# A mixer kernel on one core: TensorE's filler transposes ahead of the gated layer are taken out

## The reference, cut to what matters

```python
# attention, 4 x 8 heads, 576 x 64 each, causal, with a decaying bias
scores = scale * np.matmul(q, k.transpose(0, 1, 3, 2))
cum = np.cumsum(np.maximum(s, 0.0), axis=-1)
bias = -(cum[:, :, :, None] - cum[:, :, None, :])
scores = np.where(causal, -1e9, scores + np.minimum(bias, 0.0))
attn = softmax(scores);  x = attn @ v            # heads side by side: 576 x 512
# the gated layer: x mixed with x one token back
xk = mu_k * x + (1.0 - mu_k) * x_prev;  xr = mu_r * x + (1.0 - mu_r) * x_prev
k = np.maximum(xk @ w_k, 0.0);  v = k * k @ w_v
x = sigmoid(xr @ w_r) * v
# the mixer: over tokens, then over channels
h = np.maximum(x.T @ w_tok1, 0.0) @ w_tok2;  u = x + h.T
out = u + np.maximum(u @ w_ch1, 0.0) @ w_ch2
```

## Time and profile before

| | |
|---|---|
| median of 3 executions | 952.55 us (948.29 to 953.51) |
| the profiled execution: its own time | 947.21 us |
| its span, first to last instruction | 945.4 us |
| mean granted TensorE clock over the span | 0.987 |
| TensorE busy with matmuls | 888.6 us, 94% |
| VectorE, ScalarE, GpSimd busy | 55%, 41%, 42% |
| slots 0 to 33, up to the first product of the gated layer | about 128.5 us |

### The profile page before, as it was taken

How to read it: one execution, slowest core, us unless ns; L and a number is a source line. 1 busy time by engine, 2 the same in 40 slices (tenths; PEclk the granted TensorE clock), 3 DMA queues, 4 the chain that set the end, 5 groups by cost and what they waited for, 6 DMA issues and landing times.

```text
span 945.4 us, 18975 instructions
## 1 busy us (share of the span) xinstructions
PE 888.6 (94%) x6693; PEld 826.9 (87%) x6693; DVE 519.9 (55%) x1228; ACT 384.9 (41%) x985; POOL 396.4 (42%) x684
## 2 busy tenths in 40 slices
PE   5886789999999999999999989999999999999997
PEld 3665578889888988888899979999999999999996
DVE  3666668878878788787866743222323232323222
ACT  2575567566565666656634521211121112111110
POOL 4576986957778677776657327000000000000000
PEclk9997799999999999999999999999999999999999
DMA  7521212031320312212040240100010001000000
GB/s 243 141 85 38 64 39 64 20 95 38 89 59 24 95 39 81 61 32 70 2 184 27 76 151 9 51 26 1 25 50 25 0 25 50 25 0 26 1 26 26
DMA packets 79982, 51.62 MB, mean 55 GB/s; under 512 B 60321, under 2 KB 69089, under 8 KB 79905
## 3 DMA queue, kind: packets, MB, share of 16 engines
q1 hardware_dynamic: 79904, 50.63, 18.6%
HBM read 41.10 MB, written 9.51 MB: 54 GB/s over the span
## 4 chain that ended last, share of the span: by engine, by line
PE 72%; issue 8%; DVE 7%; POOL 6%; ACT 4%; DMA 1%; SPq 1%; DVEq 0%; POOLq 0%; ACTq 0%
PE psum L175 55%; PE psum L760 6%; PE psum L716 3%; PE psum L731 3%; POOL sq L641 2%; DVE z L1131 2%; ACT z L944 2%; POOL v_hl L564 1%; PE psum L697 1%; DVE p_t L1149 1%; PE psum L854 1%; POOL z L578 1%; POOL k_lo L645 1%; PE psum L741 1%; PE psum L834 1%
## 5 line engine op out<-in xcount | busy, mean ns | idle before, releaser
L175 PE MATMUL psum<-u_hi,c_hi 128*128 128x288 f32 x384 | 116.9, 304 | 2.8 <-DVE u_lo L1266 2.8
L1276 DVE SCALAR_TENSOR_TENSOR hid_lo<-psum,hid_hi 128x288 fp32r<-128x288 f32 x96 | 43.9, 457 | 132.7 <-ACT hid_hi L1050 132.7
L1050 ACT ACTIVATE hid_hi<-psum 128x288 fp32r<-128x288 f32 x96 | 39.4, 411 | 184.2 <-PE psum L175 184.2
L175 PE MATMUL psum<-hid_hi,c_hi 128*128 128x288 f32 x384 | 113.9, 297 | 0.0
L175 PE MATMUL psum<-u_hi,c_lo 128*128 128x288 f32 x384 | 113.7, 296 | 0.0
L175 PE MATMUL psum<-u_lo,c_hi 128*128 128x288 f32 x384 | 113.6, 296 | 0.0
L578 POOL TENSOR_SCALAR z<-cum_k,cum_qp 128x128 f32<-128x128 f32 (+4 forms) x160 | 91.7, 582 | 51.8 <-DMA cum_k<-cum_scratch 42.6
L175 PE MATMUL psum<-hid_hi,c_lo 128*128 128x288 f32 x384 | 113.3, 295 | 0.0
L175 PE MATMUL psum<-hid_lo,c_hi 128*128 128x288 f32 x384 | 113.2, 295 | 0.0
L944 ACT ACTIVATE z<-z,z_min 128x128 f32<-128x128 f32 (+4 forms) x160 | 95.1, 596 | 37.7 <-DVE z_min L1131 37.4
L1131 DVE CUSTOM_DVE_ANT_0 z<-psum,z 128x128 f32<-128x128 f32 (+4 forms) x160 | 70.5, 477 | 25.0 <-PE psum L716 17.8
(11 more groups left out here) (121 smaller groups left out, 2335.0 us busy)
## 6 DMA issues: line engine op xcount, KB each, us to landing
cum_k<-cum_scratch SPq DMA_DIRECT2D x32, 288.0 KB, 3.7
q_raw<-in_q SPq DMA_DIRECT2D x32, 144.0 KB, 2.6
k_raw<-in_k SPq DMA_DIRECT2D x32, 144.0 KB, 2.8
mixed_scratch<-gate SPq DMA_DIRECT2D x32, 144.0 KB, 1.8
x_t<-mixed_scratch SPq DMA_DIRECT2D x8, 576.0 KB, 4.4
out<-o_sb SPq DMA_DIRECT2D x24, 192.0 KB, 2.1
v_raw<-in_v SPq DMA_DIRECT2D x32, 128.0 KB, 2.5
c_raw<-in_moe_w_ch SPq DMA_DIRECT2D x4, 768.0 KB, 6.4
```

The costliest lines, as they stand in the source:

```text
L175: done = nc.tensor.matmul(out, w[a][0:r, tw, w_cols], x[b][0:r, tx, x_cols], start=first and n == 0 and m == 0, stop=last and n == len(til ...
L1050: nc.scalar.activation(hid[0][:, f % 3, :], s_bank[f % 2][:, 0:HALF], ACT.Relu).then_inc(hid_hi, 1)
L1276: nc.vector.scalar_tensor_tensor(hid[1][:, f % 3, :], s_bank[f % 2][:, 0:HALF], 0.0, hid[0][:, f % 3, :].bitcast(F32), ALU.max, ALU.subtra ...
```

## The change

One constant goes from 4 to 0. In slots 0 to 33 keep_busy() then issues nothing, so 34 times 4 transposes of 128 x 128 are gone from TensorE's list, with their weight loads. Everything else, on TensorE and on the other engines, keeps its order and its waits.

```diff
--- before.py
+++ after.py
@@ -67,7 +67,7 @@
 GATE_AT = 34
 FIRST_PAIRS, TURN_PAIRS = [0, 7, 14, 21], [-6, 4]
 PAIR_AT = FIRST_PAIRS + [GATE_AT + turn * TURN_SLOTS + at for turn in range(STEPS - 2) for at in TURN_PAIRS]
-KEEP = 4
+KEEP = 0
 LAST_SLOT = GATE_AT + STEPS * TURN_SLOTS
 TWO_LEFT = GATE_AT + (STEPS - 2) * TURN_SLOTS
 
```

## The result

The change makes the kernel slower. Its median is 963.34 us (961.28 to 967.04, 4 executions) against 950.42 (945.85 to 953.51, 4 executions); the ratio is 1.0152 with a 95% interval of 1.0114 to 1.0189. Later, in other executions beside other kernels, it was 1.0183 (1.0147 to 1.0220). The forecast of 953 and its range to 962 are both exceeded. These ratios are not the quotients of the two medians, which are 1.0136 and 1.0194.

The account below looks back on a forecast made before the run. TensorE's chain of waits and its clock were taken to bound the first 128.5 us: 4.4 us of filler back, 5.4 lost to a late first rise, +1.0 on the 952.55 median, forecast 953 us; range 946 to 962, 8 times in 10.

Parts of the forecast that it names:

- the chance of falls in the thin stretches: Between vA and w3, around q and k: perhaps a clock fall without filler; no separate price or chance.
- Rival (2): Slots 0 to 33: clock stays low for most of the stage, +18 us, 970.5; two late rises 960; chance 0.25.
- the filler's removal from the waits: Behind k, w4, s3 and w2: TensorE waits there anyway, so removing transposes costs and gives nothing; idle time becomes longer.
- The step on the first rise: Near 29 us, first pair of heads: the shortened unbroken run makes the clock rise late, costing 5.4 us from vA to vB.
- The price of the low level: First pair of heads at the lower clock: 5.4 us from vA to vB, plus 2.4 for its s-pieces.
- the filler's own time: Removed transposes on TensorE's chain up to 128.5 us: 4.4 us come back, at most 7.2, at least nothing.
- the gated layer's start: First product expected between 128 and 131 us; from there to the end the two traces should differ by nothing.
- The long x_mix of VectorE behind GpSimd's weights: 92.6 to 108 us: VectorE waits out GpSimd's weights, 2.36 us for one and 5.36 for two; no filler gain counted there.

## Why the prediction was wrong

**The step that failed is the chance of falls in the thin stretches.** Rival (2) named it ("perhaps a fall in the thinner stretch between vA and w3"), weighed it with "more than the 0.95 us in 4.0 ahead of a fall, but not by much", and gave it no price: its 22.4 us are all put down to late rises. The only falls in the trace of before had come behind nearly idle stretches, and I took these for the border. They were only examples on one side of it. The changed kernel lost its clock with 1.24 and with 1.84 us of work in 3.40; a stretch with 2.16 in 3.42 holds in the kernel before (and no new border lies between these: 2.35 fell and 1.76 held elsewhere, as shown above). What I had not done is to go through one pair and add up what is left in each wait without the filler: I had written that the filler's removal from the waits "costs and gives nothing; the idle time becomes longer", and it was exactly there that it did its work. Eight transposes at the two thinnest places alone give the time of before back (0.9987), with no filler left on the chain, though not its clock (0.964 to 0.976 over the span, against 0.977 to 0.985).

**The step on the first rise was the wrong one to forecast.** I expected it late, at 5.4 us, as the one loss. In the profiled execution it came close to 28.0 us, within an unbroken run of 4.8 us; in the other one it was missed behind a run just as long and came some 28 us later. So that it "can go either way" was right, and the mechanism exists, but the two executions lie at 962 and 967 us, not at 948 and 953.

**The price of the low level was nearly right.** The prediction's pieces make 5.4 + 2.4 = 7.8 us for one pair. Measured, a pair at the low level takes 28.6 us and one at the high level 21.1, so 7.5. In part that is luck: vB takes 2.1 us more at the low level (4.4 against 2.3), not 1.6, and s1 (1.65 against 0.96) was left out, while the wait ahead of k becomes 0.5 us shorter. By the granted clocks of the two windows up to the gated layer (0.68 of 145.92 and 0.92 of 128.53 us) the changed kernel was at the low level for some 73 us more, two and a half pairs; an estimate from these numbers is 19 us, less what the filler's own time gives back, against the 17.4 measured. The +7 to +18 us of rival (2) are where the result lies, and I had given that rival 0.25; but its price was of late rises, and that falls in the thin stretches come to as much is luck too.

**The filler's own time was put too high.** 4.4 us on the chain by the prediction; 2.6 and about 2 by the two pairs of kernels that differ in nothing else, with intervals that overlap. (The prediction also counts one piece too many behind w1: three of 0.44 us stand in the chain, at 49.07, 70.30 and 126.73. Its sum doesn't use them.) The chain of waits counts a piece in full if it was the last thing before the next. The rows of the kernel with no filler between vA and q show where the rest went: q starts earlier, but the wait between q and k grows to 1.08 us, because ScalarE isn't free for q_t any sooner (it is at the low part o_lo until 31.11 and begins q_t at 31.14). From vA to k it is 3.41 us there (32.19 - 28.78), before 3.61 by the same two rows; 0.2 of the 0.46 us came back.

**What held.** Nothing changed behind the gated layer's start but 2.4 us made up, which no run took apart. The long x_mix of VectorE behind GpSimd's weights is there in both kernels and isn't most of the loss: in the changed kernel

```profile
78.45 4.28 DVE L1202 SCALAR_TENSOR_TENSOR x_mix<-x_all,mu,x_mix 128x288 f32<-128x288 f32 x2
...
109.14 6.26 DVE L1202 SCALAR_TENSOR_TENSOR x_mix<-x_all,mu,x_mix 128x288 f32<-128x288 f32 x1
```

these three and the one between them (1.03 us at 104.74) are 11.6 us together; before, the same four took 5.36, 2.63 (at 95.98) and 2.36, 10.4 together. That may be some 1.2 us of the loss in that execution; no run took it apart.

**What stays open.** What exactly makes the clock fall is read here only from rows on either side. The spread of one program over 16 us, the two unbroken runs of 4.8 us of which one brought the rise and one didn't, and the stretches of 2.35 us that fell and of 1.76 that held, say that something beside the time at work decides. It may be the moment at which a stretch comes, or what kind of work stands in it; no run separated these. Open too is how much of the 6 us that eight in each wait gain comes from the earlier first rise and the shorter falls, and how much from the free chain.

## What to carry to other kernels

Work that nobody reads can be what keeps TensorE at its full clock, so before taking filler out, go through the stage wait by wait and add up how little is left in each; the thin ones are where the clock can go, and the waits are where filler costs least (eight transposes still fitted into the one behind k). Fill the waits and leave the chain free: the same kernel with eight transposes in each wait and none elsewhere is 0.6% faster than with four everywhere, and 2.4% faster than with none. And when one program's executions lie more than one per cent apart with the mean clock, compare medians of many, since one profile shows one course of the clock.

## What the runs showed of the hardware that was not expected

The clock fell after a stretch in which TensorE was at work for more than half of the time (1.84 of 3.40 us), with no wait longer than 1.6 us in it, and once after 2.35 of 3.40, while it held through 1.76 of 3.40 in another kernel. Of two unbroken runs of 4.8 us at the low level, one brought the rise and one didn't. fp32 transposes hold the clock as plain matmuls of the same length do (ratio to before 1.0005, 0.9969 to 1.0042).
